# Attention and two MLPs on one core: the pairs of heads evenly spaced, and the second MLP's weights prepared inside one block

## The reference

```python
# attention, for each of the 32 heads
out_d     = softmax(scale * mean4(q) @ mean4(k).T) @ mean4(v)     # 144 positions, each repeated 4 times
out_local = softmax(where(|i - j| < 4, scale * q @ k.T, -1e9)) @ v
x = (repeat(out_d, 4) + out_local) as [2304 tokens, 512]
# first MLP: 512 -> 1024 -> 512 (no nonlinearity between w3 and w_out)
h = (x @ w1) * (x @ w2);  x = (h @ w3) @ w_out
# second MLP: 512 -> 768 -> 512
h = max(max(x @ u1, x @ u2), x @ u3);  out = h @ u_out
```

## Time and profile before

| | us |
|---|---|
| median of 3 runs | 704.42 |
| the three runs | 702.22, 704.42, 706.07 |
| the profiled execution, its own time | 706.01 |
| its span, first to last instruction | 704.2 |
| PE busy | 684.6 (97%) |
| DVE, ACT, POOL busy | 376.4, 242.2, 264.5 |
| mean granted TensorE clock | 0.995 of full |

### The profile page before, as it was taken

One profiled execution on the slowest core, in us unless ns is written; L12 is line 12 of the kernel. 1 busy time (PEld: TensorE's weight loads), 2 busy tenths in 40 slices (PEclk: granted clock), 3 DMA queues, 4 the chain that ended last, 5 costly groups with the idle time before them and its releaser, 6 DMA issues.

```text
span 704.2 us, 15733 instructions
## 1 busy us (share of the span) xinstructions
PE 684.6 (97%) x6632; PEld 608.6 (86%) x6632; DVE 376.4 (53%) x705; ACT 242.2 (34%) x514; POOL 264.5 (38%) x241
## 2 busy tenths in 40 slices
PE   6999999999999999999999988999999999999998
PEld 4777788888888888888887988999999999999997
DVE  3464554414544044432665646566775667746673
ACT  5364432313332233333655544122341223403221
POOL 6799432312234023231222129043490434903341
PEclk9999999999999999999999998999999999999999
DMA  9874222111222022103998979876589765797632
GB/s 322 274 227 145 65 84 76 56 43 55 76 77 76 24 76 76 55 25 110 312 309 288 332 263 373 291 247 238 182 299 379 248 240 179 302 369 253 214 132 90
DMA packets 43798, 131.73 MB, mean 187 GB/s; under 512 B 4944, under 2 KB 8272, under 8 KB 42960
## 3 DMA queue, kind: packets, MB, share of 16 engines
q1 hardware_dynamic: 43728, 130.73, 53.7%
HBM read 103.97 MB, written 26.74 MB: 186 GB/s over the span
## 4 chain that ended last, share of the span: by engine, by line
PE 82%; DMA 6%; DVE 4%; POOL 3%; ACT 2%; issue 1%; SPq 1%; ACTq 0%; DVEq 0%
PE psum L585 25%; PE psum L587 24%; PE psum L586 24%; DMA weights_stream<-attention 4%; PE psum L624 2%; PE psum L602 2%; PE psum L595 2%; DVE attention L749 2%; POOL second_split L1147 2%; ACT attention L993 2%; DMA attention<-qk 2%; PE psum L612 1%; PE psum L633 1%; SPq L534 1%; DMA xy<-wa 1%
## 5 line engine op out<-in xcount | busy, mean ns | idle before, releaser
L585 PE MATMUL psum<-second_split,weights_split 128*128 128x384 f32 x402 | 135.7, 338 | 4.3 <-POOL second_split L1147 2.9
L586 PE MATMUL psum<-second_split,weights_split 128*128 128x384 f32 x402 | 134.9, 336 | 0.0
L587 PE MATMUL psum<-second_split,weights_split 128*128 128x384 f32 x402 | 134.9, 336 | 0.0
L1147 POOL TENSOR_TENSOR second_split<-xy,second_split 128x384 fp32r<-128x384 f32 x75 | 81.9, 1119 | 133.6 <-ACT second_split L993 133.6
L1147 POOL TENSOR_TENSOR h_split<-gate,h_split 128x512 fp32r<-128x512 f32 (+1 forms) x40 | 47.1, 1177 | 205.3 <-ACT h_split L993 205.3
L585 PE MATMUL psum<-x_split,weights_split 128*128 128x512 f32 (+1 forms) x320 | 120.4, 376 | 0.0
L587 PE MATMUL psum<-x_split,weights_split 128*128 128x512 f32 (+1 forms) x320 | 117.9, 369 | 0.0
L586 PE MATMUL psum<-x_split,weights_split 128*128 128x512 f32 (+1 forms) x320 | 117.9, 368 | 0.0
L585 PEld LDWEIGHTS psum<-second_split,weights_split 128*128 128x128 f32 x402 | 76.0, 189 | 6.6 <-issue 3.9
L586 PEld LDWEIGHTS psum<-second_split,weights_split 128*128 128x128 f32 x402 | 75.9, 189 | 0.0
L587 PEld LDWEIGHTS psum<-second_split,weights_split 128*128 128x128 f32 x402 | 75.9, 189 | 0.0
(11 more groups left out here) (101 smaller groups left out, 1152.5 us busy)
## 6 DMA issues: line engine op xcount, KB each, us to landing
weights_split<-weights_stream SPq DMA_DIRECT2D x39, 768.0 KB, 5.2
weights_split<-weights_stream SPq DMA_DIRECT2D x54, 512.0 KB, 5.0
weights_stream<-attention SPq DMA_DIRECT2D x48, 256.0 KB, 3.1
xy<-wa SPq DMA_DIRECT2D x40, 256.0 KB, 4.9
attention<-qk SPq DMA_DIRECT2D x16, 576.0 KB, 4.2
weights_stream<-attention SPq DMA_DIRECT2D x24, 384.0 KB, 2.8
weights_split<-weights_stream SPq DMA_DIRECT2D x6, 1152.0 KB, 5.0
attention<-v_win SPq DMA_DIRECT2D x16, 384.0 KB, 3.6
```

The costliest lines, as they stand in the source:

```text
L585: pe.matmul(out, lhs[:, 0], rhs[:, 0], start=first, stop=False, skip_group_check=read_between)
L586: pe.matmul(out, lhs[:, 0], rhs[:, 1], start=False, stop=False, skip_group_check=read_between)
L587: return pe.matmul(out, lhs[:, 1], rhs[:, 0], start=False, stop=last, skip_group_check=read_between)
L1147: return pool.tensor_tensor(out, full, high.bitcast(F32), ALU.subtract)
```

## The change

The positions of the attention units and of the preparations change; no instruction is added, taken away or altered, and no other function is touched.

```diff
 def position(name, u):
     ...
     if u < PAIRS:
         return FIRST_VISITS[visit][u] + late
-    return PROLOGUE + PARTS * (u // PAIRS - 1) + 11 * (u % PAIRS) + 1.5 + VISITS[visit] + late
+    return PROLOGUE + 10.4 * (u - PAIRS) + 1.5 + VISITS[visit] + late
 
 def preparations(late):
 
-    return [PROLOGUE + PARTS * 2 + (49 + 2.6 * n + late if n < 18 else 97 + 5 * (n - 18) + 2 * late) for n in range(PREPS)]
+    return [PROLOGUE + PARTS * 2 + 33.5 + 2.6 * n + late for n in range(PREPS)]
```

## The result

The changed kernel takes 696.86 us (median of 6 runs, 695.59 to 697.44) against 704.02 for the kernel before (6 runs beside it, 702.22 to 706.07). The ratio is 0.9899, 95% interval 0.9882 to 0.9917: 7.2 us faster, 1.0%. The forecast was 698.3, range 694.8 to 702.3. The profiled execution took 696.18 us, 9.83 less than the one of before.

What follows compares the result with a forecast made beforehand. PE bounds the kernel, busy 684.6 of 704.2 us. -8.0 us at the last block's end and +1.5 at block 3's boundary give -6.5 on 706.01, so 699.5; less 1.2 for the median, 698.3 us, range 694.8 to 702.3.

Steps and rivals of the forecast that it cites:

- Part one: Blocks 0 to 3: placing the pairs of heads 10.4 parts apart by itself changes the time by 0.
- The bound of 2.99 us: Attention on PE: from V's start to the end of x_out, which the next scores wait for, are 2.99 us.
- rival B: Pairs too close: scores wait for x_out eleven times, also behind a gate product; about 712 us, chance 0.05.
- The slack of 1.4 us: Between pairs: next scores come 4.4 us after V's start, x_out ends after 2.99 us; 1.4 us are left.
- Point 3: Last block's end: POOL's splits start earlier, PE's matmul behind the tenth 6.5 us earlier, at 429.65.
- Points 1 and 2: Last block's second layer: waits behind gate product 7 go, 2.7 us, and the slow clock behind them, 1.6 us.
- Point 4: Nine matmuls behind 436.16, after the tenth split: full clock in place of the slow one, 1.5 us saved.
- The cost at block 3's boundary, +1.5 us: Gate product behind preparation 17's low part, preparations falling back: +1.5 us, bounds -1.1 and +4.7.
- Rival A: DMA holds the preparations up at block 3's boundary, costing 4.7 us: 701.3 us, chance 0.18.
- 13 us before ScalarE needs them: End of the preparations: the last stores land at 402, 13 us before ScalarE needs them.

Runs made afterwards that it cites:

- e1: The changed kernel with the preparations back at their old positions, so only the pairs of heads move; 703.73 us, ratio 1.0005 against the kernel before.
- e11: The changed kernel with the pairs of heads 8.7 parts apart in place of 10.4; 703.36 us, ratio 1.0008 against the kernel before.
- e6: The changed kernel with the pairs of heads 9.0 parts apart in place of 10.4; 697.53 us, ratio 0.9901 against the kernel before.
- e8: The changed kernel with ScalarE's first y split held until the second output tile of the last block's second layer; 702.55 us, ratio 0.9981 against the kernel before.
- e2: The changed kernel with all preparations 0.1 part earlier (33.4 for 33.5); 696.98 us, ratio 0.9916 against the kernel before.
- e4: The changed kernel with all preparations 8 parts later (41.5 for 33.5); 698.38 us, ratio 0.9936 against the kernel before.
- e3: The kernel before with its first 18 preparations 0.1 part later (49.1 for 49); 701.73 us, ratio 0.9977 against the kernel before.

## Why the prediction was right, and where it was off

*Part one costs nothing.* Right: e1 at 1.0005. The bound of 2.99 us between V and x_out held to the hundredth at the three places of e11, and rival B came true at 8.7 parts, by the bare bound at three places and behind a gate product at the fourth. The slack of 1.4 us that I gave it was a little short: in e6, with one part (1.36 us) less, 0.3 us were left.

*Point 3, the splits start 6.5 us earlier.* Right in mechanism, off by the boundary term: the chain starts at 416.47, not 417.3, as the last block begins 1 us earlier, and lasts 12.27 us. 428.79 against the 429.65 forecast. The waits on the ninth and tenth split were 0.36 and 0.43 us.

*Points 1 and 2, the waits on `h_split` and the slow clock behind them.* They went as forecast (the layer took 11.52 us). But e8 shows that they were hidden: it has neither of them, and with the splits late it is only 1.2 us below the kernel before, about what block 3's boundary gives; PE only waits longer behind them. That holds for most of their size and not to the last tenth, as e8's chain starts 6.6 us after the first layer's end and that of the kernel before 8.4. e1 shows the same from the other side, 1.6 us less on `h_split`'s waits and 1.8 more on `second_split`'s. The prediction said that point 3 contains them, and added only point 4; this kept the sum right.

*Point 4, no slow clock.* Right: 1.00 in the stretch from 414.5 to 428.8. It was worth 1.3 us.

*The cost at block 3's boundary, +1.5 us.* Wrong, in sign: measured -1.1 us, the lower of the two bounds given. The step that failed is "Due every 3.53 us (2.6 x 1.36) and done every 3.80, the preparations fall back by 0.27 us each; six more of them have run by that boundary". Copies 0 to 17 of the kernel after ran from 306.39 to 367.21, 3.58 us each (6 to 17, in the first layer, from 327.60 on, 3.60), and e2, with 18 preparations up to the boundary and the old order, is as late there (2.96 us) as the kernel before with 12 (3.09). No backlog is carried from the first six. What set the lateness was which of two neighbours on VectorE comes first: 33.5 + 2.6 x 6 is 49.1, not 49. That tenth put gate product 2 ahead of the combination of preparation 10, and gate product 5 ahead of the low part of preparation 14. The prediction gave the order at position 240 alone, where nothing changes; the swaps are 8 and 20 parts earlier. Which of the two swaps does it wasn't tried.

*Rival A.* The waits of ScalarE for stores are there in the kernel after as well. The longest, 2.93 us at preparation 21, is in a second layer, where nobody waits for it. One of 1.29 us, at preparation 17, stood just where rival A put it, but PE did not wait. The Trainium skill's figure of about 358 GB/s for HBM ("DMA: Bandwidth & Descriptors", "Where 436 GB/s comes from") would have put this term at most at 0, and it is below 0. A preparation has 1.18 MB, so I had made 3.86 us of it by the 306 GB/s that I took from the trace for a ceiling, and it took 3.58; from 330 to 397 us the kernel after moved 319 GB/s. So 306 GB/s at a share of 0.88 wasn't DMA's limit. Nor is the page's figure a ceiling in this case: the kernel before moved 378 GB/s at a share of 0.94 from 423.2 to 436.6 us, and there the measurement decides.

*"13 us before ScalarE needs them".* The stores landed at 397, 18 us before. But the spare time was not to be had: e4 used up 8 parts of it and lost about 1.5 to 2.2 us. The landing was not the next limit; the place of a preparation ahead of a gate product in VectorE's queue was.

*How much of the closeness is luck.* From the profiled execution of before I took off 6.5 us; it was 9.8. Of the 3.3 us between them the boundary is 2.6 and the "issue" wait 1.0, and the other terms take back 0.3 to 0.4. Then I took off 1.2 us for the median, but the median of after lies 0.7 us above its profiled execution. The two errors have opposite signs, and 698.3 came within 1.4 us of 696.86 partly by that. The runs also tell where the spread of the kernel before lay. In the 51 executions of it beside the experiments, the 21 with a granted clock of 0.998 took 702.8 us on average and the 24 with 0.995 took 704.2, while all six of the changed kernel had 0.999 or 1.000. So part of the clock's cost was not in every execution of before, and the medians gained less than the two profiles.

## What to carry to other kernels

When a chain that sets the start of the next stage is late, waits ahead of it on the bound engine are hidden beneath it; price the chain's start and add only what lies behind it. Move bulk preparation out of a stage whose steps are short, even where its results aren't needed until later. Where the order on an engine is sorted from computed positions, compare the sorted lists over the whole stretch after a change, as a shift of a tenth can swap neighbours, and e3 gained 1.6 us (0.6 to 2.7) by that alone.

## What was unexpected of the hardware

At waits of PE of 1.34 us the granted clock fell to 1.2 GHz in all three of their places in the profiled execution of e11 (averages of 0.75, 0.72 and 0.72 over 5, 6 and 6 us). At 129.1 in the same execution PE waited 1.61 us and the clock stayed at 1.00, and in e1 it stayed at 1.00 behind a wait of 1.05 us. Such a fall costs beside the wait: with 5.6 us of waits on x_out this execution was 9.8 us longer than the profiled one of the changed kernel. It also comes and goes between executions of one kernel, as the clocks of e11's ten show (0.992 to 1.000). In the forecast I had taken 0.92 us as harmless and 2.1 as harmful. The 1.34 and 1.61 us of e11 show that the length of a wait alone doesn't decide it; what else does is open.
